# Attention and mixer kernel on one core: an order of loads in the second pair, a wait in the first, and the stores of the last batch

## The chip, the cores and the metric

The kernel runs on one core of one Trainium2 chip, as one program. The metric is the device time of the whole program in microseconds. The kernel before takes 661.63 us, the median of 3 runs (661.38 to 661.79).

## The reference, cut to what matters

```
def rotate(x):                       # rotary embedding, tables cos and sin by position
    x1, x2 = (x[..., :half], x[..., half:])
    return np.concatenate([x1 * cos - x2 * sin, x1 * sin + x2 * cos], axis=-1)
q_rot, k_rot = (rotate(q), rotate(k))            # B=4, H=8, S=576, D=64
scores = scale * np.matmul(q_rot, k_rot.transpose(0, 1, 3, 2))
scores = scores - np.max(scores, axis=-1, keepdims=True)
attn = np.exp(scores)
attn = attn / (np.sum(attn, axis=-1, keepdims=True) + 1e-09)
x = np.matmul(attn, v)                           # then laid out as (4, 576, 512)
h = np.maximum(x.transpose(0, 2, 1) @ w_tok1, 0.0) @ w_tok2    # 576 -> 256 -> 576
u = x + h.transpose(0, 2, 1)
h2 = np.maximum(u @ w_ch1, 0.0) @ w_ch2                        # 512 -> 1536 -> 512
out = u + h2
```

Everything is float32. Products are made of two parts of each operand: a rounded part ("hi") and the rest ("lo"), and two or three matmuls replace one.

## The kernel before, in words

**Two stages.** The first stage is the attention. The 32 heads are worked on as 16 pairs, head A and head B of a pair side by side in the 128 partitions. The second stage is the mixer, one batch of the 4 after another.

**Attention.** A pair has 9 tiles of queries: tiles 0 to 3 are head A's, tile 4 holds the last 64 queries of both heads, and tiles 5 to 8 are head B's. The loop of `tensor` for p = 1 to 15 weaves two pairs: it scores pair p, and turns and multiplies by v what is left of pair p-1. The text numbers pairs from 0, as the code does, so the second pair is pair 1. `score` makes 128 x 576 scores in one of two score slots; VectorE takes the row maximum (line 932), ScalarE the exponential (line 793). `turn` transposes a tile's probabilities on TensorE into a bank of the PSUM tensor `rest`; ScalarE copies the hi part out (line 800) and VectorE the lo part (line 940). `turn_tails` does the same for the last 64 keys of a group of tiles (lines 591, 808, 948). `values` multiplies by v (line 604).

**Where q and k come from.** Sync loads raw q, k and v (`load`, lines 360 to 366). GpSimd rotates them (`rotate`, lines 327 to 335), but for pair 0. TensorE transposes the rotated tiles (line 533), and ScalarE and VectorE split them (lines 780, 921, 924). From the split tiles Sync puts together, by DMAs from SBUF to SBUF, what one head's scores are made of: `assemble_k` (2 DMAs, lines 398 and 399) and `assemble_q` (3 DMAs, lines 387 to 389). The first score of a head waits until all 5 of them have landed (`tiles_in`). The raw buffers of q and k are single: `load_next("q", p + 3)` may only start once GpSimd has made its products from the q of pair p + 2 (the semaphore `products`), since it overwrites it.

**What sets the order.** Every engine runs a fixed list written out by hand, in order. On Sync, too, a DMA stands behind every wait that comes before it in the list. Head B of pair p + 1 is put together behind `load_next("q", p + 3)` in the loop of `sync`.

**Mixer.** For each batch: four `u_unit`s, 12 `hidden` products, then seven `channel` products (a scheme with seven products in place of eight), in the order of `WEIGHTS`; the last is A22, six steps of two halves g of three matmuls each (lines 1206 to 1208). VectorE adds the products up in `out_t`, which has channels in partitions; `sum_up` number 9 adds A22 to the two channel groups 2 and 3 for tokens 0 to 287. `to_rows` then transposes `out_t` into rows of tokens: part 0 is token groups 3 and 4, part 1 is groups 0 and 1, part 2 is group 2 (`ROWS`); token group t holds tokens 4p + t, and group 4 the last 64. ScalarE copies each part out of PSUM (lines 1370, 1372), and Sync stores it (lines 1176 and 1180). In the last batch nothing follows these stores; Sync waits for them to land (line 1187), and the program ends.

## Time and profile before

| | |
|---|---|
| median of 3 runs | 661.63 us |
| the profiled execution, its own time | 661.01 us |
| its span | 659.2 us |
| PE (TensorE matmul) busy | 637.5 us, 97% |
| DVE (VectorE) busy | 463.5 us, 70% |
| ACT (ScalarE) busy | 413.9 us, 63% |
| POOL (GpSimd) busy | 256.5 us, 39% |

How to read it: PEld is the loading of weights into TensorE, which runs beside the matmuls; SPq is the queue of Sync, whose instructions are DMA issues. Times in the rows are microseconds from the start of the span. The span is cut into 40 slices on the page; in the first three PE is not busy all the time (its digits there are 3, 7 and 9), and in the last neither (6). A duration of a matmul is longer than the distance to the next one, as they are pipelined: the distance is what a matmul costs. The time of the execution is 1.8 us more than its span.

### The profile page before, as it was taken

The page shows a single profiled execution, that of the slowest core. Times are in us where ns is not written, and L with a number is a line of the kernel's source. Part 1 is how long each engine was busy: PE and PEld are TensorE (multiplying, and loading weights), DVE is VectorE, ACT ScalarE, POOL GpSimd, SP SyncE. Part 2 cuts the span into 40 slices and gives each one's busy share as a digit, 9 for nine tenths or more (in the row PEclk, how much of TensorE's full clock was granted, in tenths as well). Part 3 has the DMA queues.
Part 4 walks back from the last instruction along what each step waited for, and adds up shares of the span by engine and source line. Part 5 has one row for each costly group of instructions (what it writes and reads, how often), then busy time and mean ns, then how long its engine had stood idle before and what let it go on. Part 6 is the DMA issues. An engine that isn't in the chain of part 4 may idle for free.

```text
span 659.2 us, 13577 instructions
## 1 busy us (share of the span) xinstructions
PE 637.5 (97%) x4848; PEld 620.8 (94%) x4848; DVE 463.5 (70%) x823; ACT 413.9 (63%) x923; POOL 256.5 (39%) x255
## 2 busy tenths in 40 slices
PE   3799999999999999999999999999999999999996
PEld 3789999999999999989999999999999999999996
DVE  7889999999999999976476851238820387413584
ACT  4879999988888899975464552336532255422453
POOL 4988899998888885553700000000000000000000
PEclk9999999999999999999999999999999999999999
DMA  4376756676667764406000211000310002100002
GB/s 135 101 194 182 192 150 172 178 184 170 175 177 208 201 172 115 113 19 210 1 1 1 73 32 49 1 1 2 97 56 0 0 0 80 72 1 1 1 1 73
DMA packets 59753, 59.17 MB, mean 90 GB/s; under 512 B 18736, under 2 KB 44976, under 8 KB 59696
## 3 DMA queue, kind: packets, MB, share of 16 engines
q1 hardware_dynamic: 59696, 58.42, 32.6%
q8 instruction: 35, 0.57, 0.3%
q14 instruction: 22, 0.18, 0.1%
HBM read 28.31 MB, written 9.44 MB: 57 GB/s over the span
## 4 chain that ended last, share of the span: by engine, by line
PE 93%; POOL 2%; DVE 1%; issue 1%; SPq 1%; DMA 1%; ACT 1%; ACTq 0%; DVEq 0%; POOLq 0%
PE slot L571 11%; PE rest L604 11%; PE rest L581 9%; PE slot L1206 8%; PE slot L1208 8%; PE slot L1207 8%; PE rest L1206 7%; PE rest L1208 7%; PE rest L1207 7%; PE rest L615 3%; PE rest L591 2%; PE rest L533 2%; PE slot L1238 2%; PE rest L1238 2%; PE rest L218 1%
## 5 line engine op out<-in xcount | busy, mean ns | idle before, releaser
L1436 DVE TENSOR_TENSOR pieces<-h,pieces 128x288 fp32r<-128x288 f32 x168 | 75.1, 454 | 88.6 <-ACT pieces L1358 88.3
L932 DVE TENSOR_REDUCE neg_max<-slot 128x1 f32<-128x576 f32 x142 | 106.5, 751 | 7.5 <-PE slot L571 3.1
L1358 ACT ACTIVATE pieces<-h 128x288 fp32r<-128x288 f32 x168 | 74.5, 444 | 46.5 <-PE slot L1208 28.3
L940 DVE TENSOR_TENSOR pt_lo<-rest,pt_hi 128x512 fp32r<-128x512 f32 x144 | 95.9, 677 | 1.9 <-ACT pt_hi L800 1.2
L604 PE MATMUL rest<-pt_hi,v 128*128 128x256 f32 (+1 forms) x320 | 89.4, 303 | 0.0
L800 ACT ACTIVATE pt_hi<-rest 128x512 fp32r<-128x512 f32 x144 | 84.1, 595 | 5.8 <-PE rest L581 5.2
L604 PE MATMUL rest<-pt_lo,v 128*128 128x256 f32 (+1 forms) x256 | 69.8, 295 | 0.0
L571 PE MATMUL slot<-key,q_hi 128*128 128x288 f32 x252 | 63.4, 333 | 4.3 <-ACT q_hi L835 1.5
L793 ACT ACTIVATE prob_a<-slot,neg_max 128x576 f32<-128x576 f32 x78 | 58.0, 743 | 10.0 <-DVE neg_max L932 9.6
L604 PEld LDWEIGHTS rest<-pt_hi,v 128*128 128x128 f32 x320 | 60.4, 189 | 0.2
L1449 DVE TENSOR_TENSOR h<-h 128x288 f32<-128x288 f32 x96 | 41.7, 452 | 24.8 <-ACT h L1340 24.4
L1208 PE MATMUL rest<-ut_hi,w_ch_lo 128*128 128x288 f32 x192 | 56.6, 295 | 0.0
L1207 PE MATMUL rest<-ut_lo,w_ch_hi 128*128 128x288 f32 x192 | 56.6, 295 | 0.0
L1206 PE MATMUL rest<-ut_hi,w_ch_hi 128*128 128x288 f32 x192 | 56.6, 295 | 0.0
L1206 PE MATMUL slot<-ut_hi,w_ch_hi 128*128 128x288 f32 x192 | 56.6, 295 | 0.0
L1207 PE MATMUL slot<-ut_lo,w_ch_hi 128*128 128x288 f32 x192 | 56.5, 294 | 0.0
L1208 PE MATMUL slot<-ut_hi,w_ch_lo 128*128 128x288 f32 x192 | 56.5, 294 | 0.0
L571 PE MATMUL slot<-key,q_cross 128*128 128x288 f32 x252 | 54.2, 297 | 0.0
L604 PEld LDWEIGHTS rest<-pt_lo,v 128*128 128x128 f32 x256 | 48.4, 189 | 0.0
L581 PE MATMUL rest<-ident,prob_a 128*128 128x128 f32 x320 | 45.8, 273 | 2.0 <-DVE pt_lo L940 1.3
L793 ACT ACTIVATE prob_b<-slot,neg_max 128x576 f32<-128x576 f32 x64 | 47.4, 741 | 0.4 <-DVE neg_max L932 0.4
L1340 ACT ACTIVATE h<-slot 128x576 f32<-128x576 f32 x24 | 15.7, 653 | 50.6 <-PE slot L1208 50.6
(199 smaller groups left out, 1889.9 us busy)
## 6 DMA issues: line engine op xcount, KB each, us to landing
key<-t_hi_k SPq DMA_DIRECT2D x30, 144.0 KB, 2.3
key<-t_lo_k SPq DMA_DIRECT2D x30, 144.0 KB, 2.5
raw_qk<-in_q_dram SPq DMA_DIRECT2D x16, 256.0 KB, 2.7
raw_v<-in_v_dram SPq DMA_DIRECT2D x16, 256.0 KB, 3.0
x_scratch<-x_pair SPq DMA_DIRECT2D x16, 256.0 KB, 2.1
stage_or_x<-x_scratch SPq DMA_DIRECT2D x16, 256.0 KB, 4.0
raw_qk<-in_k_dram SPq DMA_DIRECT2D x15, 256.0 KB, 2.8
q_hi<-t_hi_q SPq DMA_DIRECT2D x30, 128.0 KB, 2.4
```

The source lines that it names most:

```text
L571: mm = pe.matmul(s[:, f, 0:HALF], queries, keys[:, f * HALF:(f + 1) * HALF], start=(n == 0), stop=(n == len(passes) - 1))
L581: mm = pe.transpose(rest[:, bank, j * P:(j + 1) * P], prob[i][:, j * P:(j + 1) * P], ident[:])
L604: mm = pe.matmul(rest[:, PV_BANK[f], 0:n1 - n0], v_sb[a][:, j, :], pt[:, j, n0:n1], start=(j == 0 and pt is pt_hi), stop=(j == NG - 1))
L793: act.activation(prob[i].rearrange("p (f n) -> p f n", f=2), s[:, :, 0:HALF], ACT.Exp, bias=neg_max[p % 2][:, i:i + 1], accum_out=total[p ...
L800: act.activation(pt_hi[:, 0:G, i * P:(i + 1) * P], rest[:, bank, :].rearrange("p (j n) -> p j n", j=G), ACT.Copy).then_inc(hi_done, 1)
L932: dve.tensor_reduce(neg_max[p % 2][:, i:i + 1], slot[g if 2 <= g < 4 else g % 2][:, :, 0:HALF], AX.XY, ALU.max, negate=True).then_inc(maxe ...
L940: dve.tensor_tensor(pt_lo[:, :, cols], rest[:, bank, :].rearrange("p (j n) -> p j n", j=G), f32(pt_hi[:, 0:G, cols]), ALU.subtract).then_i ...
L1206: pe.matmul(ps, lhs[0], rhs[0], start=first, stop=False, skip_group_check=True)
L1207: pe.matmul(ps, lhs[0], rhs[1], start=False, stop=False, skip_group_check=True)
L1208: return pe.matmul(ps, lhs[1], rhs[0], start=False, stop=last, skip_group_check=True)
L1358: act.activation(pieces[:, ring(m), 0, :], source[WEIGHTS[n]][:, ft, :], ACT.Copy).then_inc(piece_hi, 1)
L1436: dve.tensor_tensor(pieces[:, ring(m), 1, :], source[WEIGHTS[n]][:, ft, :], f32(pieces[:, ring(m), 0, :]), ALU.subtract).then_inc(piece_lo, 1)
```

## The change

It has three parts.

1. In `sync`, for p = 0 only, `load_next("q", 3)` stands behind `assemble_k(1, 1)` and `assemble_q(1, 1)` instead of ahead of them.
2. In `tensor`, for p = 1 only, the turn of pair 0's tile 4 (the fifth tile) waits for the lo part of the tails of tiles 0 and 1 instead of the lo part of tile 2. The turn goes to bank 0 of `rest`, which the tails had.
3. In the mixer's last batch, part 0 of the rows is made after four of the six steps of A22. The last two steps are made for g = 0 first, then the first 256 columns (channel groups 0 and 1) of token groups 0 to 2 are transposed, then the last two steps are made for g = 1, and the other two channel groups are transposed one by one as VectorE has added them up. ScalarE copies the first 256 columns and the third 128, VectorE the last 128. Sync stores the first 256 columns of the three token groups with one DMA and the last 256 columns with another, in place of one DMA for groups 0 and 1 and one for group 2.

The first place is on Sync's queue, where pair 1 is put together and pair 3 is loaded. Before:

```order
L387 DMA q_hi<-t_hi_q 64x512
L388 DMA q_cross<-t_lo_q 64x512
L389 DMA q_cross<-t_hi_q 64x512
L360 DMA raw_qk<-in_k_dram 128x2x256
L366 DMA raw_qk<-in_k_dram 64x2x64 x2
L360 DMA raw_qk<-in_q_dram 128x2x256
L364 DMA raw_qk<-in_q_dram 64x64 x2
L398 DMA key<-t_hi_k 64x576
L399 DMA key<-t_lo_k 64x576
L387 DMA q_hi<-t_hi_q 64x512
L388 DMA q_cross<-t_lo_q 64x512
L389 DMA q_cross<-t_hi_q 64x512
```

And in the changed kernel, at the same place:

```order
L387 DMA q_hi<-t_hi_q 64x512
L388 DMA q_cross<-t_lo_q 64x512
L389 DMA q_cross<-t_hi_q 64x512
L360 DMA raw_qk<-in_k_dram 128x2x256
L366 DMA raw_qk<-in_k_dram 64x2x64 x2
L398 DMA key<-t_hi_k 64x576
L399 DMA key<-t_lo_k 64x576
L387 DMA q_hi<-t_hi_q 64x512
L388 DMA q_cross<-t_lo_q 64x512
L389 DMA q_cross<-t_hi_q 64x512
L360 DMA raw_qk<-in_q_dram 128x2x256
L364 DMA raw_qk<-in_q_dram 64x64 x2
```

The first three rows are head A of pair 1. The five DMAs of head B (398 to 389) now stand ahead of the three of the q load; no DMA is added or gone.

The second place is on TensorE at the very end, from the fifth step of A22 on. A row is a matmul; the bracket names the semaphores that it waits for. Before:

```order
L1206 MATMUL rest<-pieces,w_ch_A_0 128x288 [waits piece_lo]
L1207 MATMUL rest<-pieces,w_ch_A_0 128x288
L1208 MATMUL rest<-pieces,w_ch_A_1 128x288
L1289 MATMUL slot<-ident,out_t 128x128 [waits summed]
L1289 MATMUL slot<-ident,out_t 128x128 x3
L1289 MATMUL slot<-ident,out_t 64x128 x4
L1289 MATMUL slot<-ident,out_t 128x128 [waits summed]
L1289 MATMUL slot<-ident,out_t 128x128 x7
L1289 MATMUL rest<-ident,out_t 128x128 [waits summed]
L1289 MATMUL rest<-ident,out_t 128x128 x3
```

In the changed kernel the matmuls of A22 are lines 1221 to 1223 and the new transposes are lines 1318 and 1326:

```order
L1318 MATMUL slot<-ident,out_t 128x128 x6
L1221 MATMUL rest<-pieces,w_ch_A_0 128x288 [waits piece_lo]
L1222 MATMUL rest<-pieces,w_ch_A_0 128x288
L1223 MATMUL rest<-pieces,w_ch_A_1 128x288
L1221 MATMUL rest<-pieces,w_ch_A_0 128x288 [waits piece_lo]
L1222 MATMUL rest<-pieces,w_ch_A_0 128x288
L1223 MATMUL rest<-pieces,w_ch_A_1 128x288
L1326 MATMUL rest<-ident,out_t 128x128 [waits summed]
L1326 MATMUL rest<-ident,out_t 128x128 x2
L1326 MATMUL rest<-ident,out_t 128x128 [waits summed]
L1326 MATMUL rest<-ident,out_t 128x128 x2
```

The eight transposes of part 0 have moved ahead of the last 12 products, and six further transposes ahead of the last six. Six transposes are left behind the last product, where 20 stood before, and they are released three by three.

The third place is on TensorE where the fifth tile of pair 0 is turned, between the turn of its fourth tile and the first score of pair 1. Before:

```order
L581 MATMUL rest<-ident,prob_a 128x128 [waits exped,turned_lo_done]
L581 MATMUL rest<-ident,prob_a 128x128 x3
L581 MATMUL rest<-ident,prob_a 128x128 [waits exped,turned_lo_done]
L581 MATMUL rest<-ident,prob_a 128x128 x3
L571 MATMUL slot<-key,q_hi 128x288 [waits exped,tiles_in0]
```

In the changed kernel:

```order
L584 MATMUL rest<-ident,prob_a 128x128 [waits exped,turned_lo_done]
L584 MATMUL rest<-ident,prob_a 128x128 x3
L584 MATMUL rest<-ident,prob_a 128x128 [waits exped,tails_lo_done]
L584 MATMUL rest<-ident,prob_a 128x128 x3
L574 MATMUL slot<-key,q_hi 128x288 [waits exped,tiles_in0]
```

Nothing has moved here; the wait of the third row is another. The core of the diff:

```diff
--- before.py
+++ after.py
@@ -427,12 +427,15 @@
             if p > 0:
                 load_next("k", p + 3)
             assemble_q(0, p + 1)
-            if p == 0:
+            if p > 0:
+                load_next("q", p + 3)
+            else:
                 load_next("k", p + 3)
-            load_next("q", p + 3)
             sp.wait_ge(scores, (p + 1) * TILES)
             assemble_k(1, p + 1)
             assemble_q(1, p + 1)
+            if p == 0:
+                load_next("q", p + 3)
             if 1 <= p <= len(chunks):
                 for dst, part in chunks[p - 1][0]:
                     sp.dma_start(dst, part).then_inc(w_in[p - 1], 16)
@@ -658,7 +661,10 @@
         for p in range(1, N):
             if p > 1:
                 score(p, 0)
-            after_lo(p - 1, 2)
+            if p == 1:
+                after_tails_lo(0, 0)
+            else:
+                after_lo(p - 1, 2)
             turn(p - 1, 4, 0)
             if p == 1:
                 score(p, 0)
@@ -1130,6 +1136,8 @@
     xn = token.xn
     rows = [flat[:, rows_at + i * DM:rows_at + (i + n) * DM].rearrange("p (a n) -> p a n", a=n) for i, n in ((0, 1), (1, 2), (3, 1))]
     tail_rows = flat[:, rows_at + 4 * DM:FT * S]
+    left_rows = flat[:, rows_at + DM:rows_at + 4 * DM].rearrange("p (t n) -> p t n", t=3)
+    end_top, end_low = slot[Q[1]][:].rearrange("p a n -> p (a n)")[:, 0:3 * HC * P], slot[Q[2]]
 
     top, low = slice(0, HF), slice(HF, FT)
     left, right = slice(0, HALF), slice(HALF, S)
@@ -1148,6 +1156,7 @@
     p1_copied, p5_copied, summed = sem("p1_copied"), sem("p5_copied"), sem("summed")
     rows_done = sem("rows_done")
     stored = [sem(f"stored{n}") for n in range(3)]
+    last_columns = sem("last_columns")
 
     def t_count(b, which, f):
 
@@ -1170,7 +1179,7 @@
                 sp.wait_ge(t_done, (b + 1) * TS)
                 sp.wait_ge(piece_lo, b * PIECES + 5 * HF)
                 token.load_x(sp, b + 1)
-            for r, tiles in enumerate(ROWS):
+            for r, tiles in enumerate(ROWS[0:1] if last else ROWS):
                 sp.wait_ge(rows_done, b * 3 + r + 1)
                 whole = [t for t in tiles if t < G]
                 sp.dma_start(out[b][0:MAIN, :].rearrange("(p t) n -> p t n", t=G)[:, whole[0]:whole[-1] + 1, :],
@@ -1183,6 +1192,12 @@
         first.last_store(sp)
         for b in range(B):
             body(b, last=(b == B - 1))
+        to = out[B - 1][0:MAIN, :].rearrange("(p t) n -> p t n", t=G)[:, 0:3, :]
+        sp.wait_ge(rows_done, B * 3 - 1)
+        sp.dma_start(to[:, :, 0:HC * P], left_rows[:, :, 0:HC * P]).then_inc(stored[1], 16)
+        sp.wait_ge(rows_done, B * 3)
+        sp.wait_ge(last_columns, 1)
+        sp.dma_start(to[:, :, HC * P:DM], left_rows[:, :, HC * P:DM]).then_inc(stored[2], 16)
         for r in range(3):
             sp.wait_ge(stored[r], STORES[r] * B)
 
@@ -1279,6 +1294,39 @@
                                   [pieces[:, ring(m), i, :] for i in range(2)], ft == 0 and name in FIRST_ON_SLOT, ft == HF - 1)
                 mm.then_inc(piece_used, 1)
 
+        def last_channel(b):
+
+            n = len(WEIGHTS) - 1
+            s, w = slot[SLOT["A22"]], w2["A22"]
+            pe.wait_ge(summed, b * SUMS + 3)
+
+            def piece(ft, g):
+                m = n * HF + ft
+                pe.wait_ge(piece_lo, b * PIECES + m + 1)
+                return products(s[:, g, 0:HALF], [x[:, ft, g * P:(g + 1) * P] for x in w],
+                                [pieces[:, ring(m), i, :] for i in range(2)], False, ft == HF - 1)
+
+            for ft in range(HF - 2):
+                piece(ft, 0)
+                piece(ft, 1).then_inc(piece_used, 1)
+            to_rows(b, 0)
+            piece(HF - 2, 0)
+            piece(HF - 1, 0).then_inc(piece_used, 1)
+            for t in range(3):
+                for c in range(HC):
+                    at = (t * HC + c) * P
+                    mm = pe.matmul(end_top[:, at:at + P], out_t[:, c, t * P:(t + 1) * P], ident[:], start=(at % BANK == 0),
+                                   stop=True, is_transpose=True, skip_group_check=True)
+            mm.then_inc(unit_ready, 1)
+            piece(HF - 2, 1)
+            piece(HF - 1, 1).then_inc(piece_used, 1)
+            for g in range(HC):
+                pe.wait_ge(summed, b * SUMS + 9 + g)
+                for t in range(3):
+                    mm = pe.matmul(end_low[:, g, t * P:(t + 1) * P], out_t[:, HC + g, t * P:(t + 1) * P], ident[:],
+                                   start=(t == 0), stop=True, is_transpose=True, skip_group_check=True)
+                mm.then_inc(unit_ready, 1)
+
         def to_rows(b, r):
 
             s = slot[ROWS_ON[r]]
@@ -1297,13 +1345,16 @@
                     first.last_o(pe)
             for j in range(HIDDEN):
                 hidden(b, j, begins)
-            for n in range(len(WEIGHTS)):
+            for n in range(len(WEIGHTS) - 1):
                 channel(b, n, begins)
-            to_rows(b, 0)
-            if not last:
+            if last:
+                last_channel(b)
+            else:
+                channel(b, len(WEIGHTS) - 1, begins)
+                to_rows(b, 0)
                 token_products(b)
-            to_rows(b, 1)
-            to_rows(b, 2)
+                to_rows(b, 1)
+                to_rows(b, 2)
 
         body(0, begins=True)
         with pe.Fori(1, B - 1) as b:
@@ -1362,8 +1413,8 @@
             act.wait_ge(u_added, b * 2 + side + 1)
             act.activation(out_t[:, to[0], to[1]], slot[SLOT[name]][:, :, 0:HALF], ACT.Copy).then_inc(copied, 1)
 
-        def copy_rows(b, r, last):
-            ready(act, b, CT + HIDDEN + 1 + r + (1 if r > 0 and not last else 0))
+        def copy_rows(b, r):
+            ready(act, b, CT + HIDDEN + 1 + r + (1 if r > 0 else 0))
             s = slot[ROWS_ON[r]]
             if G in ROWS[r]:
                 for a in range(2):
@@ -1396,13 +1447,21 @@
                 token.split_hi(act, b + 1, 2)
                 act.wait_ge(piece_used, b * PIECES + 41)
                 token.split_hi(act, b + 1, 3)
-            copy_rows(b, 0, last)
+            copy_rows(b, 0)
             if not last:
                 token.split_hi(act, b + 1, 4)
                 ready(act, b, CT + HIDDEN + 2)
                 token_hi(act, slot[TOK])
-            copy_rows(b, 1, last)
-            copy_rows(b, 2, last)
+            if last:
+                ready(act, b, CT + HIDDEN + 2)
+                act.activation(left_rows[:, :, 0:HC * P], end_top.rearrange("p (t n) -> p t n", t=3),
+                               ACT.Copy).then_inc(rows_done, 1)
+                ready(act, b, CT + HIDDEN + 3)
+                act.activation(left_rows[:, :, HC * P:(HC + 1) * P], end_low[:, 0, 0:3 * P].rearrange("p (t n) -> p t n", t=3),
+                               ACT.Copy).then_inc(rows_done, 1)
+            else:
+                copy_rows(b, 1)
+                copy_rows(b, 2)
 
         body(0, begins=True)
         with act.Fori(1, B - 1) as b:
@@ -1556,9 +1615,18 @@
             sum_up(b, 8, O21, at(out_t, O21), at(u, O21))
             if not last:
                 token.split_lo(dve, b + 1, 3)
-            made(b, 6)
             so_far(b, 8)
-            sum_up(b, 9, O21, product("A22"), at(out_t, O21))
+            if last:
+                for g in range(HC):
+                    dve.wait_ge(piece_used, used(b, 6) - (HC - 1 - g))
+                    part = out_t[:, HC + g, left]
+                    dve.tensor_tensor(part, slot[SLOT["A22"]][:, g, 0:HALF], part, ALU.add).then_inc(summed, 1)
+                ready(dve, b, CT + HIDDEN + 4)
+                dve.tensor_copy(left_rows[:, :, (HC + 1) * P:DM],
+                                end_low[:, 1, 0:3 * P].rearrange("p (t n) -> p t n", t=3)).then_inc(last_columns, 1)
+            else:
+                made(b, 6)
+                sum_up(b, 9, O21, product("A22"), at(out_t, O21))
             if not last:
                 token.split_lo(dve, b + 1, 4)
                 token_lo(b + 1, slot[TOK])
```

## Rows read from the trace of the kernel before

**Rows 1.** Waits of TensorE, 20 to 50 us: engine, operation, what released it: total, times, longest.

```profile
PEld rest L581 <- DVE pt_lo L940: 1.8, 2, 1.4
PEld slot L571 <- DMA q_cross<-t_hi_q: 1.6, 1, 1.6
```

**Rows 2.** Waits of PE, 45 to 645 us.

```profile
PE slot L571 <- ACT prob_a L793: 0.6, 1, 0.6
```

**Rows 3.** Chain that ended last, 22 to 37 us: start, duration, what.

```profile
28.40 1.57 POOL by_sin L328
...
34.12 2.74 DMA q_cross<-t_hi_q
```

**Rows 4.** Timeline of PE, up to 65 us: start, duration, what, idle before.

```profile
26.94 0.66 PE L581 MATMUL rest<-ident,prob_a 128*128 128x128 f32 x4 [1.11 <-DVE pt_lo L940]
27.35 0.51 PE L571 MATMUL slot<-key,q_hi 128*128 128x288 f32 x2
...
34.77 0.77 PE L533 MATMUL rest<-ident,rot_q 128*128 128x128 f32 x5
36.90 0.53 PE L571 MATMUL slot<-key,q_hi 128*128 128x288 f32 x2 [1.37 <-DMA q_cross<-t_hi_q]
...
62.96 0.43 PE L571 MATMUL slot<-key,q_hi 128*128 128x288 f32 x2
```

**Rows 5.** Timeline of Sync's queue, up to 60 us.

```profile
24.98 0.60 SPq L389 DMA_DIRECT2D q_cross<-t_hi_q  x1
...
26.24 1.33 SPq L366 DMA_DIRECT2D raw_qk<-in_k_dram  x2
...
59.37 0.59 SPq L389 DMA_DIRECT2D q_cross<-t_hi_q  x1
```

**Rows 6.** DMA issues, 24.95 to 25.5 us: KB each, median us from issue to landing.

```profile
q_cross<-t_hi_q SPq DMA_DIRECT2D x1, 128.0 KB, 2.3
```

**Rows 7.** Tile q_cross, whole span.

```profile
DMA to landing us min/median/max: 2.3/2.4/4.4
```

**Rows 8.** Timeline of DVE and of ACT around 25 and 35 us.

```profile
25.14 0.42 DVE L948 TENSOR_TENSOR pt_hi<-rest,pt_hi 64x256 fp32r<-64x256 f32 x1
...
36.49 0.82 DVE L921 SCALAR_TENSOR_TENSOR t_lo_q<-rest,t_hi_q 128x640 fp32r<-128x640 f32 x1
...
34.80 0.20 ACT L793 ACTIVATION_READ_ACCUMULATOR prob_a<-slot,neg_max 128x1 f32 x1
...
39.26 0.38 ACT L808 ACTIVATE pt_hi<-rest 64x256 fp32r<-64x256 f32 x1 [2.26 <-PE rest L591]
```

**Rows 9.** Timeline of all engines, 645 us to the end.

```profile
649.55 0.30 PE L1206 MATMUL rest<-pieces,w_ch_A 128*128 128x288 f32 x1
...
651.01 0.30 PE L1208 MATMUL rest<-pieces,w_ch_A 128*128 128x288 f32 x1
...
651.34 0.76 DVE L1471 TENSOR_TENSOR out_t<-rest,out_t 128x576 f32<-128x576 f32 x1 [1.46 <-PE rest L1208]
...
652.21 0.77 ACT L1370 ACTIVATE h<-slot 64x256 f32<-64x256 f32 x2 [4.39 <-PE slot L1289]
...
652.99 1.51 ACT L1372 ACTIVATE h<-slot 128x512 f32<-128x512 f32 x2
653.08 0.60 PE L1289 MATMUL rest<-ident,out_t 128*128 128x128 f32 x4
...
655.15 1.07 SPq L1176 DMA_DIRECT2D out_dram<-h  x2
```

**Rows 10.** Line 1176 (the stores of rows), 600 us to the end.

```profile
L1176 SPq DMA_DIRECT2D out_dram<-h x3: 332/442/584, 653.6 to 655.8; - x3
...
DMA to landing us min/median/max: 2.0/2.9/3.0
```

**Rows 11.** Stretches: PE, PEld, DVE, ACT, POOL busy, PEclk, DMA share, GB/s.

```profile
655.50:656.00 0.50, 0.00 (x0) 0.00 (x0) 0.00 (x0) 0.00 (x0) 0.00 (x0) 1.00 0.38 92
656.50:657.00 0.50, 0.00 (x0) 0.00 (x0) 0.00 (x0) 0.00 (x0) 0.00 (x0) 1.00 1.01 401
```

## Prediction

> **What bounds the kernel now.** I read the waits of TensorE first. Of the 659.2 us span PE is busy for 637.5; between 45 and 645 us it waits once, for 0.6 us [rows 2]. So time is to be had only where PE stands still: at the beginning, and after its last product. At the beginning the waits name two that the change speaks to: the weights of a score wait 1.6 us for the landing of q_cross, the last of five DMAs that put a head together, and a turn waits for VectorE's pt_lo (two such waits, 1.8 in all, the longest 1.4) [rows 1]. The chain through the first of them reads, backwards: DMA q_cross landed at 34.12 + 2.74 = 36.86, issued by Sync behind the load of pair 3's q, which waited for GpSimd's by_sin to end at 28.40 + 1.57 = 29.97 [rows 3]. At the end one sees PE's last product at 651.01, VectorE, transposes, ScalarE's copies, and two stores from 655.15 and 655.8, the last landing 3.0 us later, at 658.8 [rows 9, 10].
>
> **Part 1, Sync's order.** Before, Sync has issued the k load by 26.24 + 1.33 = 27.57 [rows 5], then stands until 29.97 for GpSimd. In the changed kernel the five DMAs of head B go out at once. Before, the last of the five is issued at 34.12, and the q load's first can go at 29.97 at the earliest; its three DMAs and the first four of head B fill the 4.15 us between, 0.59 each. So the fifth is now issued at about 27.6 + 4 x 0.62 = 30.1, and lands at 30.1 + 2.74 = 32.8; with the longest landing of a q_cross, 4.4 [rows 7], at 34.5.
>
> What is late next? PE starts five transposes at 34.77 [rows 4]. Their row of 0.77 is four distances and one full duration of 0.27, so a distance is 0.125 and the next work can start 5 x 0.11 to 0.125 later, at 35.32 to 35.40. Before, it started at 36.90 [rows 4]. The score needs the exponential of pair 1's fourth tile, which ends at 34.80 + 0.20 = 35.00 [rows 8]. It is free to start at 35.32, and the gain is 1.58; the wait of 1.6 [rows 1] says the same. If the fifth DMA needed all of 4.4 us, 34.5 would still be in time.
>
> Does the gain reach the end? VectorE has t_lo_q until 36.49 + 0.82 = 37.31, and PE comes to the turn into that bank at about 37.4, by my count of the rows ahead: just in time. ScalarE stood for 2.26 us ahead of 39.26 [rows 8], waiting for PE; now it stands for 0.7 and follows. From there PE's row of work is the same, and PE waits nowhere until 645 [rows 2], so what is gained stays, unless something that does not follow PE comes late (a rival below). The moved q load goes out at 30.7 instead of 29.98, lands about 0.7 later, and GpSimd, which is busy with pair 2 and v until then and with pair 3's k after, needs it only when pair 3's k is rotated: nothing. Its bounds: 0, or 0.7 if GpSimd were waiting for it. Taken: **-1.58**, between 0 and -1.6.
>
> **Part 2, the fifth tile's turn.** It waited until 26.94, 1.11 us by the row [rows 4]. VectorE's tails end at 25.14 + 0.42 = 25.56 [rows 8], so the turn now follows the fourth one at about 25.6, 1.3 us earlier. Behind it stands the first score of pair 1, which waits for head A: its last q_cross was issued at 24.98 [rows 5] and landed 2.3 later [rows 6], at 27.28. Before, that score started at 27.35 [rows 4]. So a wait of equal end stands behind the one removed: PE stands ahead of the score instead of ahead of the turn. Upper bound 1.3, if the landing did not matter; lower bound 0, since nothing comes later. I take the landing's row, 27.28 against 27.35 less the 0.04 that a wait takes to be seen (36.86 to 36.90): **0**, at most 0.1.
>
> **Part 3, the end, on the clock of the trace of before.** A22 has 36 matmuls; step five begins at 649.55 and the twelfth of the last twelve at 651.01, so the distance is 1.46 / 11 = 0.133 and the products end at 651.14 [rows 9]. A transpose costs (0.60 - 0.27) / 3 = 0.11 [rows 9]. Now: eight transposes of part 0 from 649.55 to 650.44; six products to 651.23; six transposes to 651.90; six products to 652.69, the last started at 652.56. VectorE starts 0.33 after the start of a last product (651.01 to 651.34), at 652.89. Its 288 columns for one g cost between half of the 576-column row, 0.38, and all of it, 0.76 [rows 9]; since 640 columns take 0.82 [rows 8], 64 columns are 0.06, and I take 0.76 - 4.5 x 0.06 = 0.49. It is done at 653.38. Three transposes: 0.16 to the first one's start, 2 x 0.11, and 0.27 to the end: 654.03. VectorE's copy of 384 columns likewise: 0.76 - 3 x 0.06 = 0.58, to 654.6 with the wait. Sync sees it at 654.65. ScalarE is not in the way: its two copies of 0.77 and the one of part 0 (the row of two is 1.51 for 512 and 1024 columns, so 0.6 and 0.9) run from 650.7 to 652.0; the 768 columns, ready at 652.1, are copied by 652.9, the third 128 by 653.85.
>
> Sync: part 0 with its tails takes three DMAs, 653.6 to 655.15 before, so 652.03 to 653.55 now; the first column store goes at 653.55, the second at 654.65. Before, the two stores went at 655.15 and 655.8. Both ways they carry 768 KB, and it took 3.65 us from the first issue to the last landing. By transfer alone that gives 653.55 + 3.65 = 657.2; by issue, 654.65 and a landing of 2.0 to 3.0 [rows 10] is 656.7 to 657.7. I take 657.4, near the longer landings, since both the long ones had another store ahead: **-1.4**. For the worse end: the pieces are now 1 KB long instead of 2 and 4. The stretch at 655.50, where the tails' 1 KB pieces end, moved 92 GB/s at a share of 0.38, so 242 at full share, against 401 at 656.50 [rows 11]. 786 KB at 242 instead of 401 are 1.3 us more: 658.6, a gain of 0.2. For the better end: 656.9, just before the transfer bound, a gain of 1.9.
>
> The Trainium skill, "DMA: Bandwidth & Descriptors", section "Why small descriptors are slow (HBM only)", speaks against shorter pieces: about 3 cycles are lost on each packet beside one for every 32 bytes. By that a 1 KB piece pays 3 in 35 and a 4 KB piece 3 in 131, and the two stores would take some 0.13 us more, an estimate from that page. It leaves the sum at -1.3 in place of -1.4; the trace can't separate the two, since the stretch at 242 is one in which the queue also ran dry.
>
> **The sum.** -1.58 + 0 - 1.4 = -3.0. The profiled execution took 661.01 (span 659.2), so its counterpart is 658.0 with a span of 656.2. The median of the runs is 0.6 above it, and the sum is put on the median: 661.63 - 3.0 = **658.6**.
>
> **Rivals.**
> - *A head lands late for a PE that is ahead.* Head A of pair 3 is issued last at 59.37 [rows 5] and lands 2.3 later, 61.7; its score starts at 62.96 [rows 4], which becomes 61.38. If Sync were no earlier at all, PE would stand 0.3; Sync's list should move up by some 0.8. For the rival: one q_cross took 4.4 [rows 7]; were it this one, 63.8 less 0.8 would be waited for and the 1.58 be lost. Against: it happened once in 30. Time 661.63 - 1.4 = 660.2.
> - *The end gives little*, since short pieces are slow: 661.63 - 1.58 - 0.2 = 659.9. For it the row of 242, against it that the tails' two DMAs were all that was queued there.
> - *Part 2 pays in full*: the score did not wait for head A. Then 658.6 - 1.3 = 657.3. Against: the two times agree to 0.07.
> - *Slower: stores of 1 KB pieces crawl.* One mechanism, in the last 5 us. It decides from the point where the two stores lose the 1.58 of part 1 as well: landing after 660.4, so about 0.5 earlier for the data, which are 786 KB from 654.4 to 659.9, or 143 GB/s. At the 92 of the row [rows 11] they need 8.5 us, landing at 663.4: 661.63 + 4.6 - 1.58 = 664.7. Against: 92 is at a share of 0.38.
> - *The change doesn't do what it says*: head B could be held by something else than its place in the list. Sync's wait ahead of it is for the scores of pair 0, and those are made by 27.35, when pair 1's first one starts [rows 4]. Then only the end gains: 660.2, as in the first rival.
>
> **How the numbers follow.** The forecast has 0.66 (657.9 to 659.3 by itself), the first rival and the last 0.12 together, the end giving little 0.10, part 2 in full 0.04, slower 0.03, and 0.05 is left for a loss of both gains that I can't place. About 0.2% (1.3 us) is what a measurement of this kernel can tell from no change, so faster begins below 660.3. The cases at 660.2 lie on that line, and half of them count as no change. Faster 0.87, same 0.10, slower 0.03. The range takes in 657.3 and 660.2: 657.4 to 660.3.
>
> **What would show it.** Right: no wait for q_cross in the second pair, pair 1's fifth to sixth score 1.6 us earlier, and the same 1.6 at every later place of PE up to 645; PE standing over a microsecond ahead of pair 1's first score, named for a DMA of head A, with the score still at 27.3; the last store issued some 1.1 us after the first column store and landing 7.9 us after the start of A22's fifth step, where it was 9.2. Wrong: a new wait of PE for tiles in pairs 2 to 4; a GB/s of the last stretch far below 400; a first score of pair 1 ahead of 27.

## The result and the profile after

| | before | changed |
|---|---|---|
| median | 662.33 us (8 runs, 661.38 to 664.17) | 659.48 us (8 runs, 659.05 to 660.09) |
| profiled execution, its own time | 661.01 | 659.61 |
| its span | 659.2 | 657.8 |

The ratio is 0.9953, with a 95% interval from 0.9938 to 0.9967: 3.1 us faster (2.2 to 4.1); the two medians of the table differ by 2.85. The forecast was a gain of 3.0. Its time of 658.6 lies 0.9 too low, most of which is the level of before: that kernel's median was 661.63 in the first three runs, and 662.2 to 662.7 in all later sets.

The two profiled executions differ by only 1.4 us in their spans. The lateness below is the start of a row of TensorE less the start of the same row in the trace of before; minus means earlier:

| place | row starts | lateness |
|---|---|---|
| first scores of pair 0 | 18.00, 18.59 | +0.59 |
| first score of pair 1 | 27.35, 27.91 | +0.56 |
| head B's score in pair 1 | 36.90, 35.88 | -1.02 |
| head A's score in pair 3 | 62.96, 62.30 | -0.66 |
| end of the attention | 345.12, 344.65 | -0.47 |
| first batch of the second stage | 385.14, 385.01 | -0.13 |
| all the rest, up to | 600.06, 599.93 | -0.13 |
| last landing of a store | 658.7, 657.3 | -1.4 |

The 0.59 at the beginning stands ahead of everything that the change touches (below, under the hardware). Part 1 gives 1.58 between 27 and 37 us, as the prediction has it, and part 3 gives 1.27 at the end, where it has 1.4; 0.9 is lost between 37 and 385. TensorE's timeline of the changed kernel, the rows that answer to [rows 4] (start, duration, what, idle before):

```profile
25.75 1.11 PE L584 MATMUL rest<-ident,prob_a 128*128 128x128 f32 x8 [0.22 <-DVE pt_lo L946]
27.91 0.53 PE L574 MATMUL slot<-key,q_hi 128*128 128x288 f32 x2 [1.05 <-DMA q_cross<-t_hi_q]
...
35.36 0.77 PE L536 MATMUL rest<-ident,rot_q 128*128 128x128 f32 x5
35.88 0.51 PE L574 MATMUL slot<-key,q_hi 128*128 128x288 f32 x2
...
62.30 0.52 PE L574 MATMUL slot<-key,q_hi 128*128 128x288 f32 x2 [0.27 <-DMA q_cross<-t_hi_q]
```

The row at 25.75 holds the turns of the fourth and the fifth tile (x8). Its wait of 0.22 is the fourth tile's, which before has too:

```profile
25.17 0.66 PE L581 MATMUL rest<-ident,prob_a 128*128 128x128 f32 x4 [0.22 <-DVE pt_lo L940]
```

The fifth tile, which waited 1.11, now follows without a wait. The score behind it waits 1.05 for head A: the wait has moved. At 35.88 there is no wait any more, and the score follows the five transposes by 0.52. The last row is a wait that before did not have. Sync's queue of the changed kernel, which answers to [rows 5]:

```profile
28.25 0.56 SPq L398 DMA_DIRECT2D key<-t_hi_k  x1
28.85 0.60 SPq L399 DMA_DIRECT2D key<-t_lo_k  x1
29.49 1.64 SPq L387 DMA_DIRECT2D q_hi<-t_hi_q  x1
31.17 0.60 SPq L388 DMA_DIRECT2D q_cross<-t_lo_q  x1
31.81 0.60 SPq L389 DMA_DIRECT2D q_cross<-t_hi_q  x1
32.45 0.59 SPq L360 DMA_DIRECT2D raw_qk<-in_q_dram  x1
```

The fifth DMA of head B goes at 31.81, not at the 30.1 of the prediction: the start was 0.6 later, and the issue at 29.49 stood for 1.64 instead of 0.59. It landed at 34.16, which was soon enough all the same. Waits of TensorE from 45 to 645 us, beside [rows 2]:

```profile
PE slot L574 <- ACT prob_a L799: 0.6, 1, 0.6
PE slot L574 <- DMA q_cross<-t_hi_q: 0.3, 1, 0.3
PE slot L1337 <- DVE out_t L1530: 0.2, 1, 0.2
```

The last microseconds, all engines, beside [rows 9] (at 649.42 part 0's rows stand, where before had the fifth step of A22):

```profile
649.42 1.03 PE L1337 MATMUL slot<-ident,out_t 128*128 128x128 f32 x8
...
651.95 0.81 ACT L1457 ACTIVATE h<-slot 128x768 f32<-128x768 f32 x1
652.77 0.46 DVE L1623 TENSOR_TENSOR out_t<-rest,out_t 128x288 f32<-128x288 f32 x1 [0.95 <-PE rest L1223]
653.28 0.55 PE L1326 MATMUL rest<-ident,out_t 128*128 128x128 f32 x3 [0.22 <-DVE out_t L1623]
653.43 0.59 SPq L1197 DMA_DIRECT2D out_dram<-h  x1
653.87 0.56 DVE L1625 COPY h<-rest 128x384 f32<-128x384 f32 x1 [0.64 <-PE rest L1326]
654.50 0.39 SPq L1200 DMA_DIRECT2D out_dram<-h  x1
```

Both stores landed 2.8 after their issue, the last at 657.34: 7.92 after 649.42. Before, the last landing was at 658.74, so 9.19 after 649.55 (the 658.8 of the prediction is 655.8 + 3.0, two rounded numbers). The gain is 1.27. The stretches, beside [rows 11] (busy times, granted clock, DMA share, GB/s), show the short pieces: the engines are full, and move 330 to 350 GB/s where before they moved 401.

```profile
655.00:655.50 0.50, 0.00 (x0) 0.00 (x0) 0.00 (x0) 0.00 (x0) 0.00 (x0) 1.00 1.02 330
655.50:656.00 0.50, 0.00 (x0) 0.00 (x0) 0.00 (x0) 0.00 (x0) 0.00 (x0) 1.00 1.04 350
656.00:656.50 0.50, 0.00 (x0) 0.00 (x0) 0.00 (x0) 0.00 (x0) 0.00 (x0) 1.00 1.02 348
```

### The profile page after: what moved, and what is told of

Its sections match the earlier page's. It is cut to its first block, busy times and chain, and to the rows that moved or that the text cites. A ratio compares the mean times of both kernels' runs of the same rounds, so it can differ in the third digit from the quotient of the medians.

```text
span 657.8 us, 13582 instructions
## 1 busy us (share of the span) xinstructions
PE 638.4 (97%) x4848; PEld 621.7 (95%) x4848; DVE 464.2 (71%) x825; ACT 413.4 (63%) x923; POOL 256.3 (39%) x255
## 4 chain that ended last, share of the span: by engine, by line
PE 88%; SPq 5%; DVE 2%; DMA 2%; ACT 1%; issue 1%; DVEq 0%; ACTq 0%
PE slot L574 11%; PE rest L607 10%; PE rest L584 8%; PE slot L1221 7%; PE slot L1223 7%; PE slot L1222 7%; PE rest L1223 6%; PE rest L1221 6%; PE rest L1222 6%; PE rest L618 3%; PE rest L536 2%; PE slot L1253 2%; PE rest L594 2%; PE rest L1253 2%; PE rest L215 1%; PE rest L218 1%
## 5 line engine op out<-in xcount | busy, mean ns | idle before, releaser
L1391 ACT ACTIVATE h<-rest 128x576 f32<-128x576 f32 x24 | 15.6, 650 | 50.4 <-PE rest L1223 50.4
```

## The experiments

**Each part alone.** The first kernel is before with the hunk of `sync` alone, the second with the wait of the fifth tile alone, the third with all of the rest (the last batch), the fourth the changed kernel without the fifth tile's wait.

```diff
 # fourth, against the changed kernel
-            if p == 1:
-                after_tails_lo(0, 0)
-            else:
-                after_lo(p - 1, 2)
+            after_lo(p - 1, 2)
```

> Part 1 alone (Sync's order), the rest as before. The theory of the prediction: 1.6 us faster than before less whatever a late landing gives back, so ratio 0.9976 to 0.9985; in the trace pair 1's sixth tile is scored without a wait for q_cross, 1.02 + 0.4 to 1.6 us closer to pair 1's first score than before (8.0 us after it instead of 9.55). Rival: the whole change gains at the end alone and the gain of part 1 is given back at the later waits seen in the changed kernel; then the ratio is 1.000 and TensorE waits for tiles again in pairs 2 to 4.

> Part 2 alone (the fifth tile's turn). The theory: 0 us, ratio 1.000 within its interval; TensorE waits for q_cross ahead of pair 1's first score in place of pt_lo ahead of the turn, and from the last score of pair 0 to the first of pair 1 it is the same distance as before, 4.4 us, within 0.1. Rival (part 2 pays in full): 1.3 us faster, ratio 0.998.

> Part 3 alone (the end). The theory: 1.4 us faster, ratio 0.9979, from the fifth step of A22 to the end 8.3 us instead of 9.7 (span's end). Rival (short pieces crawl): ratio 0.9997 or above, with the two last stores landing 3.3 us or more after their issue.

> The changed kernel with part 2 undone (parts 1 and 3). The theory: the same time as the changed kernel, 3.0 us below before, ratio 0.9955. If part 2 took part in the gain (by 1.3 us), the ratio is 0.9975.

| kernel | median us | ratio to before, 95% |
|---|---|---|
| part 1 | 660.51 (12 runs) | 0.9968 [0.9955, 0.9981] |
| part 2 | 663.31 (12) | 1.0016 [1.0001, 1.0030] |
| part 3 | 661.02 (12) | 0.9976 [0.9959, 0.9994] |
| parts 1 and 3 | 658.94 (6) | 0.9943 [0.9924, 0.9962] |

Part 1 gives 2.1 us, part 3 gives 1.6, both together 3.8, and part 2 nothing. The trace says the same of part 2 more sharply, since the distance from pair 0's last score to pair 1's first is free of what came before: 27.35 - 22.95 = 4.40 before, 28.27 - 23.88 = 4.39 in parts 1 and 3, 28.47 - 24.11 = 4.36 in part 2 alone and 27.91 - 23.54 = 4.37 in the changed kernel. It is worth 0.03. The kernel of part 2 measured 1.1 us slower by its median, and its interval just leaves out 1. Part of that goes with the clock, of which more below: 6 of its 12 executions had a mean granted clock of 0.996 or less, against 14 of before's 58. The other six took 662.6 on average, where before's took 662.1. Whether part 2 itself makes the lower clock more frequent is not shown.

In part 1's own trace the score of the sixth tile starts 7.97 after pair 1's first (9.55 before), as expected. The wait that it removes was not the same in every execution: in the four traces that keep Sync's old order unchanged it was 1.37 (before), 0.78 (part 2), 2.00 (part 3) and 2.31 (short pieces, below). So the 1.58 is one execution's figure. In part 3's own trace the way from part 0's rows to the end of the span is 8.39, where 8.3 was expected and before had 9.66 from the fifth step.

Part 3's own trace also brought what none of the theories had. Head B's score waited 2.00 for q_cross, and some matmuls later TensorE's rows stood 0.27 apart instead of 0.14:

```profile
38.85 0.53 PE L571 MATMUL slot<-key,q_hi 128*128 128x288 f32 x2 [2.00 <-DMA q_cross<-t_hi_q]
39.22 0.42 PE L571 MATMUL slot<-key,q_cross 128*128 128x288 f32 x2
39.48 0.31 PE L604 MATMUL rest<-pt_hi,v 128*128 128x320 f32 x1
39.63 0.31 PE L604 MATMUL rest<-pt_lo,v 128*128 128x320 f32 x1
...
40.35 0.47 PE L604 MATMUL rest<-pt_lo,v 128*128 128x320 f32 x1
40.62 0.47 PE L604 MATMUL rest<-pt_hi,v 128*128 128x320 f32 x1
```

Its stretches of 2 us give the granted clock (the number ahead of the DMA share):

```profile
38.00:40.00 2.00, 1.15 (x8) 1.15 (x9) 0.94 (x2) 0.32 (x2) 1.86 (x3) 1.00 0.68 193
40.00:42.00 2.00, 2.00 (x10) 1.87 (x9) 0.44 (x1) 0.00 (x0) 2.00 (x2) 0.51 0.89 230
```

The clock is at its lower level, 1.2 GHz, behind the standstill: at 1.00 up to 40 us and close to half of full speed in the stretch that follows. Beside the wait 1.6 us are lost (the lateness goes from 1.95 to 3.55). So the wait that part 1 removes can have a second price.

**That second price, provoked.** Before, with head B held back:

```diff
             sp.wait_ge(scores, (p + 1) * TILES)
+            if p == 0:
+                sp.wait_ge(v_split, 2)
             assemble_k(1, p + 1)
```

> The kernel before, in which Sync issues the two k copies of pair 1's head B only once pair 1's v has been split, so head B comes later than before. In one execution of the kernel with the parts' stores alone TensorE stood 2.0 us for q_cross in pair 1, and behind that standstill its matmuls stood 0.27 us apart instead of 0.14 for about 3 us, 1.6 us lost beside the wait. Theory (a longer standstill alone gives this): the wait for q_cross in pair 1 grows from 1.4 to some 3 us, rows at half the rate follow it, and the time is 662.2 + 1.9 + 1.6 = 665.7. Rival (the rows at half the rate come from something of that execution and not from the wait): only the wait counts, 664.1, with distances of 0.14 behind it.

Measured: 665.46 (7 runs), ratio 1.0042 [1.0026, 1.0058]. TensorE and its stretches in this kernel:

```profile
39.02 0.85 PE L573 MATMUL slot<-key,q_hi 128*128 128x288 f32 x2 [2.93 <-DMA q_cross<-t_hi_q]
39.66 0.68 PE L573 MATMUL slot<-key,q_cross 128*128 128x288 f32 x2
```

```profile
38.00:40.00 2.00, 0.98 (x4) 0.98 (x5) 0.00 (x0) 0.00 (x0) 1.86 (x3) 0.59 0.84 197
40.00:42.00 2.00, 2.00 (x9) 2.00 (x8) 0.76 (x1) 0.00 (x0) 2.00 (x2) 0.50 0.78 169
42.00:44.00 2.00, 2.00 (x10) 1.87 (x10) 0.38 (x1) 0.70 (x2) 1.92 (x4) 0.50 0.69 196
44.00:46.00 2.00, 2.00 (x14) 1.98 (x13) 1.01 (x3) 1.49 (x4) 1.53 (x2) 0.71 0.85 180
```

The theory holds. The lateness is 2.12 at 39.02 and 4.97 at 45.55: 2.85 lost at the lower clock behind a wait of 2.93. The stretch from 38 to 40 reads 0.59, less than a clock that fell only at 39.02 could give, so it had fallen during the standstill. The mean granted clock of each execution hints at how often it happens:

| executions | mean clock 0.996 or less |
|---|---|
| before | 14 of 58 |
| part 2, part 3 and the kernel of short pieces below, which keep the wait | 10 of 34 |
| the kernel with the wait lengthened | 6 of 7 |
| the nine sets of kernels with part 1 | 0 of 58 |

The 0.996 is a cut and not a detector. Part 3's profiled execution, which lost the 1.6 us, reads 0.997; and a clock that falls in the last microseconds, when TensorE has no work left, lowers the mean at no cost (with head A early, below, the stretch from 655 to 656 reads 0.50). Part 1 alone, which has before's end, had none in 12.

Before's 14 took 663.8 on average and its other 44 took 662.1. By that, 14/58 of 1.7, or 0.4 us of the mean, would be a gain of part 1 that the trace of before could not show, since its profiled execution had a clock of 1.000. That is an estimate: which of the 14 lost their time at pair 1 no trace says. Part 1 measured 2.1 and not 1.58; the clock can be the reason, and so can a wait that is longer than 1.37 in other executions (the four above average 1.6), and the interval of 1.25 to 3.0 takes in 1.58 itself. A standstill of 2.31 in the execution of the short pieces did not bring the clock down, one of 2.00 did; what decides between them stays open.

**Head A earlier.** If part 2 gives nothing because head A lands late, an earlier head A should set it free. For pair 1 the q copies that need only the hi part go out ahead of the wait for the lo part:

```diff
-            sp.wait_ge(t_lo_done["q"], p + 1)
+            if p == 1:
+                sp.wait_ge(t_hi_done["q"], p + 1)
+            else:
+                sp.wait_ge(t_lo_done["q"], p + 1)
```

and q_cross<-t_hi ahead of q_cross<-t_lo; once on the changed kernel, once with the fifth tile's old wait. The changed kernel was run again beside them.

> The changed kernel, in which head A's (and head B's) copies of the rounded q of pair 1 are issued as soon as ScalarE has made them, so that the last DMA of head A is the lo part and goes out some 0.2 to 0.6 us earlier. The theory that part 2 is worth nothing because head A's landing stands behind it: now the wait for q_cross ahead of pair 1's first score is shorter by that much, and the way from the last score of pair 0 to the first of pair 1 is 3.8 to 4.2 us instead of 4.36; in the time 0.2 to 0.5 us less than the changed kernel, ratio 0.995. Rival (something else sets that score): the distance stays 4.36.

> The same with part 2 undone. The theory: the turn's wait for pt_lo is the bound again, the distance is 4.40 as before and head A's earlier landing gives nothing; ratio as the changed kernel's, 0.9953. Rival: the distance is as short as in the kernel with part 2, which would say that part 2 isn't needed even then.

> The changed kernel once more, on the same chip as the three above. Every theory: ratio 0.995, and the trace tells which of its differences to the first one (start of the first transposes at 7.7, the length of the slow stretch up to 18.6, the wait for tiles in pair 3, the lost 0.3 us in the mixer's first batch) belong to the kernel and which to one execution.

Medians: 659.1 (5 runs, 0.9956 [0.9942, 0.9969]), 659.4 (5, 0.9953 [0.9940, 0.9967]), and the changed kernel 658.73 (5, 0.9943 [0.9929, 0.9956]). The edit did not do what it was for: the last of head A's copies was issued at 25.53 instead of 25.56, since Sync's five issues of 0.6 are the limit, and the distance between the two scores became 4.30 with a wait of 0.99 for q_cross<-t_lo, not the 3.8 to 4.2 expected. With the old wait it is 28.84 - 24.45 = 4.39. So both ends, pt_lo and the landing, stand within 0.1 us of each other, and to take away either alone gave at most that. Where head A is earlier by a microsecond was not tried.

The trace of the changed kernel run again tells what belongs to the kernel and what to one execution. The slow stretch at the beginning is there again (lateness 0.81 at 18 us), and so is the loss at 385 us (1.25, below). The wait for tiles in pair 3 is not.

**Pair 3's late landing.** In the changed kernel the q_cross of pair 3's head A was issued at 58.11 and landed 4.1 later, and TensorE, ahead by 1.0, had to wait. Moved:

```diff
-            if p > 0:
+            if p > 0 and p != 2:
                 load_next("k", p + 3)
             assemble_q(0, p + 1)
+            if p == 2:
+                load_next("k", p + 3)
```

> The changed kernel, but after pair 2 Sync puts together head A's q of pair 3 ahead of the load of pair 5's k instead of behind it. In the trace of the changed kernel TensorE, which is there 1.6 us earlier, waited 0.3 us for the q_cross of pair 3's head A, which had been issued at 58.1 us and landed only 4.1 later; in the kernel with Sync's order alone it waited 0.2. Theory (there the landing is just in time, and each late landing costs): no wait for q_cross in pair 3, and what TensorE has gained at 36 us stands unchanged at 345; 0.2 to 0.4 us in one execution, so 659.2 where the changed kernel has 659.5. Rival (the landing was late because of something else in the queues, at whatever time): a wait of 0.2 or more stays in pair 3, and the time is the changed kernel's.

Measured: 658.4 (6 runs), 0.9937 [0.9918, 0.9956]. The copy is issued at 56.20, and there is no wait for q_cross in pair 3; the lateness of -1.18 at 36 us is still -1.21 at 55 and -1.49 at 345, where the changed kernel has -1.05 and -0.47. The theory holds in this trace, but the trace alone does not decide: of the six other traces with part 1 and the old order in pair 3, only two had the wait (the changed kernel 0.27, part 1 alone 0.20), and four had none. What speaks for the edit is its slack: issued at 56.20, even a landing of 4.1 would be there at 60.3. The time is below that of the changed kernel, but its interval takes that in. What delayed the landing shows in the transfers of the changed kernel from 59 to 59.5 us (queue: packets, MB, share of 16 engines):

```profile
q1 hardware_dynamic: 63, 0.10, 83.9%
q8 instruction: 1, 0.02, 19.1%
```

An instruction fetch in one packet took 19.1% of 16 engines for 0.5 us, so one of them for 1.5 us. The longest landing of before, 4.4 [rows 7], coincides with one too (issued at 46.76, the fetch at 48.0 to 48.5 with 18.8%). All 14 traces of this case say the same. They hold 840 of these copies. Of the 647 with no instruction fetch of 8 or 16 KB between issue and landing, none took over 2.58 us. Of the 193 with one, 112 took longer than that, up to 4.46. So every long landing has a fetch beside it, though not every fetch makes one. No run moved a fetch, so this is a regularity and not an experiment. The late landings also come at like places: 13 of the 14 traces have one over 3.5 us near 132 to 139 or 218 to 225 us.

**All that the traces suggested.** To the above come two edits that the second stage asked for. In its first batch TensorE loses time after a late reload of x. ScalarE's wait for it in four traces, in the order before, changed, part 1 alone, the changed kernel again:

```profile
ACT x_parts L198 <- DMA stage_or_x<-x_scratch: 0.4, 1, 0.4
```

```profile
ACT x_parts L198 <- DMA stage_or_x<-x_scratch: 0.8, 1, 0.8
```

```profile
ACT x_parts L198 <- DMA stage_or_x<-x_scratch: 2.0, 1, 2.0
```

```profile
ACT x_parts L198 <- DMA stage_or_x<-x_scratch: 1.7, 1, 1.7
```

TensorE's loss at 385 us was 0, 0.34, 1.53 and 1.25; with the exact waits of 0.42, 0.78, 1.97 and 1.69 it is each time the wait less 0.42 to 0.44. With head A early, under either wait of the fifth tile, ScalarE waited at most 0.36 and nothing was lost, so the loss comes with the execution and not with every early TensorE. That reload took 8.3 to 9.9 us from its first issue to ScalarE's start in these four, whether TensorE is early or late; before stood just at the edge, where a wait of 0.42 costs nothing. Kernels with the old order can lose in the same way, at the reload for the next batch: part 2 alone and part 3 alone waited 0.76 and 0.83 there, at 471 and 474 us, and lost some 0.5. Two kernels were made: the first has the head A and pair 3 edits and the last 128 columns copied by VectorE (256 elements) and ScalarE (128); the second also issues the reload's tails first and the last batch's tail stores behind the first column store.

> A version meant to beat both: the changed kernel with head A's copies early, with pair 3's q put together ahead of the k load of pair 5, and with the last 128 columns copied out by VectorE (two token groups) and ScalarE (one). The theory: no wait for tiles in pair 3 (0.3 us in the changed kernel's trace), 0.3 us at pair 1, and VectorE's last copy 0.43 instead of 0.56 us, so 0.1 at the end: 0.7 us less than the changed kernel, ratio 0.994. Rival: the waits move to the next landing and the ratio stays 0.9953.

> The changed kernel with all that its trace suggests: pair 1's head A without waiting for the lo part at its first copies, pair 3's q ahead of pair 5's k, the last 128 columns copied by VectorE and ScalarE together, and, new, two edits on Sync: the reload of x for the next batch issues its two tail DMAs first, and the last batch's two tail stores go behind the first column store. Theory: in the traces so far TensorE loses, in the first batch of the second stage, what ScalarE waits for the reload of x less 0.43 us (waits of 0.42, 0.78, 1.09, 1.69 and 1.97 gave losses of 0, 0.34, 0.68, 1.25 and 1.53), and the last DMAs to land are the tails'. Issued first, they no longer end last, so the wait for x is at most 0.43 and nothing is lost at 385 us; the first column store is issued 0.6 earlier, and the last landing comes 0.2 to 0.3 earlier. 658.3, where the same kernel without these two had 658.7. Rival (what lands last is a single late packet of whichever DMA, and the last stores are bound by their transfer from the moment the last one can start): waits over 0.43 stay possible, the last landing does not move, 658.7.

Measured: 658.67 (5 runs, 0.9946 [0.9932, 0.9959]) and 658.68 (6 runs, 0.9938 [0.9920, 0.9956]). Neither can be told from the changed kernel. In the second ScalarE still waited 0.72 for x, so the order of the tails is not what makes it late, and that half of the theory falls. At the end, the time from part 0's rows to the last landing was 7.92 in the changed kernel, 655.62 - 647.69 = 7.93 in the first and 656.33 - 648.61 = 7.72 in the second. In the first the last store went 0.93 behind the first column store instead of 1.07, and nothing landed sooner. In the second the first column store went at 651.96, 3.35 after part 0's rows (4.01 in the changed kernel), but the tails behind it held the last one until 653.63; the landing came 0.2 sooner, as the theory had it, which the median can't show. The end is one transfer, as the rival says: what counts is when the first large store can go.

**What short pieces cost.** Before, with the last batch's token groups 0 to 2 stored in two column halves, both behind all rows; the last store carries 384 KB in 1 KB pieces.

```diff
-            for r, tiles in enumerate(ROWS):
+            for r, tiles in enumerate(ROWS[0:1] if last else ROWS):
 ...
+        sp.wait_ge(rows_done, B * 3)
+        sp.dma_start(to[:, :, 0:HC * P], left_rows[:, :, 0:HC * P]).then_inc(stored[1], 16)
+        sp.dma_start(to[:, :, HC * P:DM], left_rows[:, :, HC * P:DM]).then_inc(stored[2], 16)
```

> The kernel before, with the last batch's rows of groups 1 to 3 stored as two column halves of 1 KB pieces once all rows are there, instead of as one row group of 2 KB and two of 4 KB pieces... The computation and the order of everything ahead of the stores are those of before; only the pieces are shorter and the first of the two stores waits for the last rows. Theory (pieces of 1 KB run at the 330 to 350 GB/s of the changed kernel's last stretches against 401): stretches at full share show 330 to 350 GB/s, and 786 KB take 0.3 us more than at 401. The wait of the first store for the last rows costs 0.5 more, so 663.0. Rival (the rate in the changed kernel was lowered by something else at its end, such as part 0's tails): the stretches show 400.

Measured: 662.2 (10 runs), 1.0001 [0.9985, 1.0018]. Its stretches:

```profile
657.00:657.50 0.50, 0.00 (x0) 0.00 (x0) 0.00 (x0) 0.00 (x0) 0.00 (x0) 1.00 1.03 328
657.50:658.00 0.50, 0.00 (x0) 0.00 (x0) 0.00 (x0) 0.00 (x0) 0.00 (x0) 0.91 1.04 358
658.00:658.50 0.50, 0.00 (x0) 0.00 (x0) 0.00 (x0) 0.00 (x0) 0.00 (x0) 0.50 1.04 346
```

The rate is the pieces' own, 328 to 358 GB/s at full share. The two column stores on Sync's queue, and the time from the second one's issue to its landing:

```profile
655.72 0.59 SPq L1189 DMA_DIRECT2D out_dram<-h  x1
656.35 0.52 SPq L1190 DMA_DIRECT2D out_dram<-h  x1
DMA to landing us min/median/max: 3.3/3.3/3.3
```

The second landed at 659.63. Less this execution's lateness of 0.57 that is 659.06, where before had 658.74. Both stores went at the same moments as before's two (less the 0.57, 655.15 and 655.78). So the short pieces cost 0.3, as the theory has it for the rate; the median, with an interval of over 1 us to either side, can't show it. My 0.5 for the wait was wrong: Sync was busy with the tails until then in any case.

From the first of the two large stores to the last landing the traces give only two values. With 2 and 4 KB pieces it is 3.57 to 3.59 (before, part 1, part 2, head B later). With 1 KB pieces it is 3.90 to 3.93 in nine traces, whether the last store was issued 0.63, 0.93 or 1.07 behind the first. So the end of the changed kernel is bound by this transfer, and not by the issue of the last store.

## Why the prediction was right

- *Part 1, -1.58.* Right in the trace to 0.01 (+0.56 to -1.02), for the reason given: the transposes are the next thing late. The runs give 2.1 [1.25 to 3.0]. The difference can be chance, a wait that is longer in other executions (0.78 to 2.31 in four traces), or the lower clock behind it, put at 0.4 in the mean by the estimate above. The prediction had neither the spread of the wait nor the clock.
- *The q load moved back* cost nothing, as said: pair 3's head A, whose q it brings, was put together by a last copy issued at 58.11, where before issued it at 59.37. The new wait for a tile in pairs 2 to 4, which the prediction named as a sign of being wrong, did come once, with 0.27 in pair 3; it is the late landing told below.
- *Part 2, 0.* Right: 4.40 became 4.37. PE stood 1.05 ahead of the score, named for head A's DMA. The score started at 27.91 and not at 27.3, since all of the execution was 0.6 later.
- *Part 3, -1.4.* Right in kind and 0.1 too large: 7.92 to the last landing, 9.19 before, so 1.27, and the same within 0.03 in the traces of part 3 alone, parts 1 and 3, and the changed kernel run again. The last store went 1.07 behind the first (1.1 was said). VectorE's addition took 0.46 (0.49 worked out) and its copy 0.56 (0.58). The prediction set two bounds side by side, 657.2 by transfer from the first store and 657.4 by issue and landing of the last, and took the second. The first is the one that binds: it took 3.91 and not 3.65, as the pieces are shorter, and so it ends about where the other was put. That the sum came out within 0.1 is in this part luck. Alone, part 3 measured 1.6 [0.4 to 2.7].
- *"The same 1.6 at every later place of PE up to 645."* This failed. 0.39 went at pair 3, 0.18 in small steps up to 280, and 0.34 at 385 (the 0.2 that TensorE waits for out_t in the list beside [rows 2] is there, at 385.01). The first is the first rival, in its mild form: the landing of 4.1 came with pair 3's head A, and TensorE lost 0.4 and not 1.58. Its reason against, "once in 30", read only the longest landing of [rows 7]: the trace of before has a second of the kind, 4.15 for the copy issued at 220.21. The last had no place in the prediction, which asked what q_cross can do to a TensorE that is ahead, and not what the reload of x can. In parts 1 and 3, and in the changed kernel run again, the loss at 385 was 0.68 and 1.25, and that at pair 3 was nothing.
- *The price of short descriptors.* The sum held nothing for it at the middle. The stretches show a lower rate (330 to 358 against 401), and the kernel of short pieces landed 0.3 later with nothing else moved. The prediction's estimate by the Trainium skill, "DMA: Bandwidth & Descriptors", section "Why small descriptors are slow (HBM only)", was 0.13: the right way, and less than half of what the traces show. The rival of crawling pieces is out.
- *The chances.* Added up as described they give 0.86 for faster and 0.11 for the same, where the text has 0.87 and 0.10.

The misses, part 1 with more than 1.58 by the runs and up to 0.9 of it lost again on the way, pull in opposite directions. So that the sum of 3.0 lies within 0.15 of what was measured is partly luck.

## What to carry to other kernels

A wait of the engine that bounds the kernel costs its length, and perhaps the clock behind it (seen in one trace at a standstill of 2.0 us and in one at 2.9; of the seven executions of the latter kernel six had a low mean clock); look at the mean clock of many executions and not at the one that was profiled. A gain stays a gain only as far as the next transfer that does not follow the engine: list all of them (here the heads, and the reload of x 340 us later) with the slack of each, and take the longest landing seen and not the median. Where two releasers end within 0.1 us of each other, to remove one is worth the 0.1.

## What the runs showed of the hardware that was not expected

- Behind a standstill of TensorE of 2.93 us its matmuls ran at the lower clock from 39.0 to some 45 us (0.50 in the stretches between 40 and 44), and 2.85 us were lost; one of 2.00 cost 1.6, one of 2.31 nothing, and that of 1.37 in the profiled execution of before nothing.
- The first scores of pair 0 run at double distance (0.46 to 0.48 between rows instead of 0.26), as at the lower clock level. It ended at 17.2 us before and at 18.6 in the changed kernel, which alone is 0.6 us:

```profile
17.17 0.68 PE L574 MATMUL slot<-t_hi_k,t_hi_q 128*128 128x288 f32 x2
17.65 0.68 PE L574 MATMUL slot<-t_lo_k,t_hi_q 128*128 128x288 f32 x2
18.13 0.62 PE L574 MATMUL slot<-t_hi_k,t_lo_q 128*128 128x288 f32 x2
18.59 0.43 PE L574 MATMUL slot<-key,q_hi 128*128 128x288 f32 x2
```

  The granted clock of these stretches is printed as 1.00, but that is no measurement. The clock records in the traces begin only at 17.17 us before and at 18.54 in the changed kernel, where the distances halve, and a stretch without a record is printed as 1.00. In the 14 traces the first record comes between 16.2 and 19.6 us. No run shows what sets the moment.
- The start varies by itself: TensorE's first transposes began between 7.60 and 8.56 us in traces of kernels that are the same up to there.
- A 128 KB copy from SBUF to SBUF lands after 2.4 us in the median. It took over 2.58 us in 112 of 840 cases, up to 4.46, and each time an instruction fetch ran beside it.
- Stores in 1 KB pieces filled the DMA engines at 328 to 358 GB/s, in pieces of 2 and 4 KB at 401; the last 768 KB took 3.9 us from first issue to last landing instead of 3.6.
